# First attention pair: a bias scanned on two partitions and spread by TensorE, loads in three parts, the full scan behind the first logits, ten products before the work

## The reference

```python
# q, k, v: (4, 8, 576, 64); s: (4, 8, 576)
scores = scale * q @ k.T                        # scale = 1/8
s_pos = np.maximum(s, 0.0)
cum = np.cumsum(s_pos, axis=-1)
bias = -(cum[..., :, None] - cum[..., None, :])
scores = np.where(causal, -1e9, scores + np.minimum(bias, 0.0))
attn = softmax(scores);  x = attn @ v           # (2304, 512)
x = ((x @ w_in) * cos(x @ w_in)) @ w_out        # d_ff 2048
out = gated block of rms_norm(x)                # d_ff 1536
```

## Time and profile before

| | us |
|---|---|
| median of 3 runs | 1067.96 (1067.79 to 1068.59) |
| the profiled execution, its own time | 1068.27 |
| its span in the trace | 1066.5 |
| PE busy | 1047.6 (98%) |
| DVE busy | 590.5 (55%) |
| ACT busy | 484.3 (45%) |
| POOL busy | 274.3 (26%) |

### The profile page before, as it was taken

The page is one execution under the profiler, slowest core; times in us unless marked ns, Lnnn a source line. Parts: engine busy times, 40 slices in busy tenths (PEclk is TensorE's granted clock), DMA queues, the critical chain, the costliest instruction groups (busy, mean ns, idle before and its releaser), DMA issues.

```text
span 1066.5 us, 16586 instructions
## 1 busy us (share of the span) xinstructions
PE 1047.6 (98%) x6116; PEld 996.7 (93%) x6116; DVE 590.5 (55%) x1148; ACT 484.3 (45%) x1030; POOL 274.3 (26%) x216
## 2 busy tenths in 40 slices
PE   5999999999999999999999999999999999999998
PEld 4998999899999999999999999999999999999997
DVE  6888888698555655556567644334334334433322
ACT  5888887655554555545546422222222222322211
POOL 5898896575000000000042794000000000000000
PEclk9999999999999999999999999999999999999999
DMA  6654542143000000000011241000000000000000
GB/s 205 200 183 140 170 154 94 54 133 114 2 1 1 1 1 0 0 0 0 0 48 32 89 119 40 30 1 1 30 0 0 30 0 0 30 0 0 30 1 30
DMA packets 23368, 52.35 MB, mean 49 GB/s; under 512 B 3920, under 2 KB 3920, under 8 KB 23312
## 3 DMA queue, kind: packets, MB, share of 16 engines
q1 hardware_dynamic: 23312, 51.62, 15.1%
HBM read 46.74 MB, written 4.87 MB: 48 GB/s over the span
## 4 chain that ended last, share of the span: by engine, by line
PE 93%; DVE 4%; ACT 1%; DMA 1%; issue 1%; POOL 0%; SPq 0%; DVEq 0%; ACTq 0%; POOLq 0%
PE psum L1231 28%; PE psum L1215 17%; PE psum L1155 16%; PE psum L1257 14%; PE psum L1105 7%; PE psum L1136 5%; PE psum L1118 4%; DVE b_r L789 1%; PE psum L1109 1%; DVE b_r L786 1%; DMA raw<-in_qkv 1%; DVE b_lo L827 0%; DVE b_g L822 0%; DVE w L867 0%; DVE first_sq L839 0%
## 5 line engine op out<-in xcount | busy, mean ns | idle before, releaser
L1231 PE MATMUL psum<-c_x,cw 128*128 128x384 f32 x1728 | 313.1, 335 | 0.0
L1231 PEld LDWEIGHTS psum<-c_x,cw 128*128 128x128 f32 x1728 | 303.3, 188 | 6.1
L1215 PE MATMUL psum<-b_hi,w 128*128 128x384 f32 x768 | 211.0, 335 | 4.1 <-DVE b_lo L827 4.1
L1215 PEld LDWEIGHTS psum<-b_hi,w 128*128 128x128 f32 x768 | 140.0, 188 | 5.2 <-DVE b_lo L827 5.0
L929 DVE TENSOR_TENSOR c_t<-psum,c_t 128x384 f32<-128x384 f32 x72 | 40.1, 557 | 186.6 <-ACT c_t L673 186.1
L1257 PE MATMUL psum<-cw,c_hi 128*128 128x512 f32 x432 | 136.2, 396 | 0.1
L673 ACT ACTIVATE c_t<-psum 128x384 f32<-128x384 f32 x72 | 35.4, 492 | 207.4 <-PE psum L1231 206.1
L1215 PE MATMUL psum<-b_lo,w 128*128 128x384 f32 x384 | 128.3, 334 | 0.0
L1105 PE MATMUL psum<-qk 128*128 128x192 f32 (+6 forms) x480 | 99.4, 337 | 11.3 <-DVE qk L716 8.8
L1155 PE MATMUL psum<-bx_even,w 128*128 128x384 f32 x576 | 108.0, 335 | 0.0
L1155 PE MATMUL psum<-bx_odd,w 128*128 128x384 f32 x576 | 107.5, 334 | 0.0
(11 more groups left out here) (92 smaller groups left out, 1473.3 us busy)
## 6 DMA issues: line engine op xcount, KB each, us to landing
raw<-in_qkv SPq DMA_DIRECT2D x15, 864.0 KB, 4.4
stage<-in_w_out SPq DMA_DIRECT2D x28, 256.0 KB, 2.6
raw<-in_qkv SPq DMA_DIRECT2D x16, 320.0 KB, 3.2
inv_row<-inv_rows SPq DMA_DIRECT2D x32, 144.0 KB, 3.4
out<-stage SPq DMA_DIRECT2D x18, 256.0 KB, 2.1
cum<-cum_rows SPq DMA_DIRECT2D x30, 144.0 KB, 3.2
stage<-in_w_in SPq DMA_DIRECT2D x16, 256.0 KB, 2.7
stage<-in_w_gate SPq DMA_DIRECT2D x12, 256.0 KB, 2.6
```

The source lines that it names most:

```text
L1215: last = mm(Y_BANKS[f][:, 0:TB], out1_w(j, a)[:, cols], g[j % 2][:], start=(j == 0 and m == 0), stop=(j == NJ - 1 and m == 2))
L1231: last = mm(to[:, 0:TC], weights(c, a)[:, kc], c_x[:, b, kc], start=(kc == 0 and m == 0), stop=(kc == KC - 1 and m == 2))
```

## The change

The bias of pair 0 is no longer broadcast by DMA. ScalarE's queue loads the two rows of `s` onto two partitions and then all of `s`. VectorE clips and scans the two rows there, into `x_part[0:2]`. GpSimd makes one more constant, `spread` (2 x 128, row 0 is one in columns 0 to 63, row 1 in 64 to 127), in three more instructions. TensorE multiplies `spread` by the scanned rows in two float32 products of 288 columns, so that all 128 partitions have their head's row, and ScalarE copies that from PSUM to `cum8[0]`.

Pair 0 is loaded and split in three parts of 704, 384 and 640 columns, pair 1 in two of 832 and 896. The v of pair 0 is loaded behind pair 1. On VectorE the casts of the constants come before the bias; the full scan and the third low split stand behind the logits of tile 0. TensorE begins with ten 128-column products of ones that nothing reads.

```diff
+FIRST_QK = [0, SEQ + P, SEQ + 4 * P, QK_COLS]
+FIRST_TILES = [0, 1, 4]
+SECOND_QK = SEQ + 2 * P
+WARM_UP = 10
-        CONSTS_POOL = 9
+        CONSTS_POOL = 12
# SP queue
-            for a in range(2):
-                sp.dma_start(cum8[1][HALF_ROWS[a], :], s_h[a:a + 1, :].to_broadcast([64, SEQ])).then_inc(s_first_loaded, 16)
-            for n, (lo, hi) in enumerate(((0, FIRST_QK), (FIRST_QK, QK_COLS), (QK_COLS, PAIR_COLS))):
+            for n in range(3):
+                lo, hi = FIRST_QK[n:n + 2]
                 sp.dma_start(raw[0][:, lo:hi], qkv[0, :, lo:hi]).then_inc(first_loaded[n], 16)
-            sp.dma_start(s_sb[:], s_h).then_inc(s_loaded, 16)
-            load_qk(1)
+            sp.dma_start(raw[1][:, 0:SECOND_QK], qkv[1, :, 0:SECOND_QK]).then_inc(second_loaded, 16)
+            sp.dma_start(raw[1][:, SECOND_QK:QK_COLS], qkv[1, :, SECOND_QK:QK_COLS]).then_inc(qk_loaded[1], 16)
+            sp.dma_start(raw[0][:, QK_COLS:PAIR_COLS], qkv[0, :, QK_COLS:PAIR_COLS]).then_inc(first_v_loaded, 16)
             load_v(1)
# ScalarE
+            act.dma_start(cum8[1][0:2, :], s_h[0:2, :]).then_inc(s_first_loaded, 16)
+            act.dma_start(s_sb[:], s_h).then_inc(s_loaded, 16)
             first_split_hi(0)
             first_split_hi(1)
+            act.wait_ge(first_spread, 1)
+            nc.scalar.copy(cum8[0][:, :].rearrange("p (a n) -> p a n", a=2),
+                           psum[:, 2:4, 0:HALF8]).then_inc(first_cum, 1)
+            first_split_hi(2)
# VectorE: the scan on 128 partitions before the casts goes, and behind the casts stands
+            dve.wait_ge(s_first_loaded, 16)
+            nc.vector.tensor_scalar(cum8[1][0:2, :], cum8[1][0:2, :], 0.0, 1.0 / SCORE_SCALE, ALU.max, ALU.mult).then_inc(first_pos, 1)
+            dve.wait_ge(first_pos, 1)
+            nc.vector.tensor_tensor_scan(x_part[0:2, :], ones_f[0:2, 0:1].to_broadcast([2, SEQ]), cum8[1][0:2, :], 0.0,
+                                         ALU.mult, ALU.add).then_inc(first_scan, 1)
             first_split_lo(0)
             first_split_lo(1)
             dve.wait_ge(s_loaded, 16)
             nc.vector.tensor_scalar(s_sb[:], s_sb[:], 0.0, 1.0 / SCORE_SCALE, ALU.max, ALU.mult).then_inc(spos_ready, 1)
-            dve.wait_ge(spos_ready, 1)
-            nc.vector.tensor_tensor_scan(cum[:], ...).then_inc(cum_ready, 1)
             dve.wait_ge(first_cum, 1)
...
                 do(0, logits, 0)
+                if t == 0:
+                    all_cum()                    # the same scan
+                    first_split_lo(2)
# GpSimd: pair 1 in two parts
+                parts = ((0, SECOND_QK), (SECOND_QK, QK_COLS)) if p == 1 else ((0, QK_COLS),)
# TensorE
+            pe.wait_ge(consts_dve, 1)
+            for _ in range(WARM_UP):
+                mm(bank[7][:, 0:P], ones_f[:], ones_f[:], start=True, stop=True)
             pe.wait_ge(consts_pool, CONSTS_POOL)
             pe.wait_ge(consts_dve, CONSTS_DVE)
+            pe.wait_ge(first_scan, 1)
+            for a in range(2):
+                last = mm(bank[2 + a][:, 0:HALF8], spread[:], x_part[0:2, a * HALF8:(a + 1) * HALF8], start=True, stop=True)
+            last.then_inc(first_spread, 1)
```

More of the change, by code:

```diff
@@ L120, in fused_kernel @@
                 ident = sb("ident", [P, P], F32, sA)
+                spread = sb("spread", [2, P], F32, sA)
                 ident_b = sb("ident_b", [P, P], BF16, sA)
@@ L204, in fused_kernel @@
         first_loaded = [sem(f"first_loaded{i}") for i in range(3)]
+        first_v_loaded = sem("first_v_loaded")
+        second_loaded = sem("second_loaded")
+        first_scan = sem("first_scan")
+        first_spread = sem("first_spread")
         first_hi = sem("first_hi")
@@ L388, in load_qk @@
                 if p == 2:
-                    sp.wait_ge(first_lo, 2)
+                    sp.wait_ge(first_lo, 3)
                 elif p > 2:
-                    at_least(sp, qk_lo, p - 2)
+                    at_least(sp, qk_lo, p - 1)
                 sp.dma_start(raw[p % 2][:, 0:QK_COLS], qkv[p, :, 0:QK_COLS]).then_inc(qk_loaded[p % 2], 16)
@@ L403, in load_cum @@
                 else:
-                    sp.wait_ge(first_cum, 1)
+                    sp.wait_ge(first_scan, 1)
                 for a in range(2):
@@ L712, in first_split_lo @@
             def first_split_lo(n):
-                lo, hi = ((0, FIRST_QK), (FIRST_QK, QK_COLS))[n]
+                lo, hi = FIRST_QK[n:n + 2]
                 at_least(dve, first_hi, n + 1)
@@ L722, in _, with all_cum @@
             nc.vector.tensor_scalar(s_sb[:], s_sb[:], 0.0, 1.0 / SCORE_SCALE, ALU.max, ALU.mult).then_inc(spos_ready, 1)
-            dve.wait_ge(spos_ready, 1)
-            nc.vector.tensor_tensor_scan(cum[:], ones_f[0:NH, 0:1].to_broadcast([NH, SEQ]), s_sb[:], 0.0,
-                                         ALU.mult, ALU.add).then_inc(cum_ready, 1)
             dve.wait_ge(first_cum, 1)
+            def all_cum():
+                dve.wait_ge(spos_ready, 1)
+                nc.vector.tensor_tensor_scan(cum[:], ones_f[0:NH, 0:1].to_broadcast([NH, SEQ]), s_sb[:], 0.0,
+                                             ALU.mult, ALU.add).then_inc(cum_ready, 1)
             def logits(p, n):
@@ L969, in _ @@
                                           pattern=[[-1, P]], channel_multiplier=1))
+            const(nc.gpsimd.memset(spread[:], 1.0))
+            const(nc.gpsimd.affine_select(out=spread[:], in_=spread[:], compare_op=ALU.is_ge, fill=0.0, base=0,
+                                          pattern=[[1, P]], channel_multiplier=-HD))
+            const(nc.gpsimd.affine_select(out=spread[:], in_=spread[:], compare_op=ALU.is_ge, fill=0.0, base=HD - 1,
+                                          pattern=[[-1, P]], channel_multiplier=HD))
             for i in range(0, QT, 2):
@@ L977, in split_qk @@
                 b = p % 2
[L978 to L985, removed]
+                parts = ((0, SECOND_QK), (SECOND_QK, QK_COLS)) if p == 1 else ((0, QK_COLS),)
+                for n, (lo, hi) in enumerate(parts):
+                    if p == 1 and n == 0:
+                        pool.wait_ge(second_loaded, 16)
+                    else:
+                        at_least(pool, qk_loaded[b], 16 * ((p + 1) // 2))
+                    if p >= 2:
+                        at_least(pool, scores_done, QT * (p - 1))
+                    nc.gpsimd.tensor_scalar(qk[b][:, 0, lo:hi], raw[b][:, lo:hi], 1.0, 0.0,
+                                            ALU.mult, ALU.add).then_inc(qk_hi, 1)
+                    at_least(pool, qk_hi, p + 1 if p > 1 else n + 1)
+                    nc.gpsimd.tensor_tensor(qk[b][:, 1, lo:hi], raw[b][:, lo:hi], qk[b][:, 0, lo:hi].bitcast(F32),
+                                            ALU.subtract).then_inc(qk_lo, 1)
             def split_v(p):
@@ L990, in split_v @@
                 if p == 0:
-                    at_least(pool, first_loaded[2], 16)
+                    at_least(pool, first_v_loaded, 16)
                 else:
@@ L1085, in _ @@
             mm = nc.tensor.matmul
+            pe.wait_ge(consts_dve, 1)
+            for _ in range(WARM_UP):
+                mm(bank[7][:, 0:P], ones_f[:], ones_f[:], start=True, stop=True)
             pe.wait_ge(consts_pool, CONSTS_POOL)
             pe.wait_ge(consts_dve, CONSTS_DVE)
+            pe.wait_ge(first_scan, 1)
+            for a in range(2):
+                last = mm(bank[2 + a][:, 0:HALF8], spread[:], x_part[0:2, a * HALF8:(a + 1) * HALF8], start=True, stop=True)
+            last.then_inc(first_spread, 1)
             def scores(p, n):
                 i = TILE[n]
[L1094 to L1097, removed]
+                if p == 0 and n in FIRST_TILES:
+                    pe.wait_ge(first_lo, FIRST_TILES.index(n) + 1)
+                elif p == 1 and n in (0, 2):
+                    pe.wait_ge(qk_lo, 1 if n == 0 else 2)
+                elif p > 1 and n == 0:
+                    pe.wait_ge(qk_lo, p + 1)
                 at_least(pe, logits_ready, QT * p + (n - 1 if n >= 2 else n))
```

8 lines of the change are left out of this document (1 added, 7 removed).

## The result

The changed kernel took 1071.08 us (median of 9 executions, 1070.52 to 1072.66), the kernel before 1068.98 us (9 executions, 1067.79 to 1071.07). The ratio is 1.0021, 95% interval 1.0011 to 1.0031: about 2.1 us slower. The forecast of 1067.1 and its range up to 1069.6 were both missed, on the slow side. The profiled execution took 1070.56 us with a span of 1068.5, against 1068.27 and 1066.5: 2.0 of the 2.3 us lie inside the span. The kernel before had 1067.96 as its median of three when the forecast was made, and 1068.98 here, so 1.0 of the 4.0 us between forecast and result lies in the base.

The account below looks back on a forecast made before the run. VectorE's list, not TensorE's products, was taken to pace the opening. Of 2.2 us gained at tile 1's logits, waits beside GpSimd take back 2.0; with the clock 0.9 us is left, giving 1067.1 us, range 1065.0 to 1069.6.

Parts of the forecast that it names:

- the turns: Opening: VectorE's two-operand SBUF work and GpSimd's instructions exclude each other; waits of 1.1 + 0.9 us take back 2.0 of 2.2.
- two-row scan: Opening, VectorE: the scan of pair 0's two bias rows would be done at 6.65, against 6.77 before.
- the spread: Opening, TensorE: two float32 products of 288 columns would take 1.2 us at 2.4 GHz, 2.2 us at 1.2.
- Tile 0's logits: Opening, pair 0: they would start at 9.0 to 9.3 us, against 11.81 before.
- pair 1 landed late enough: Opening loads: pair 1's first part was taken to land at 7.8 us, between 7.1 at full rate and 8.5.
- I take them to leave it at 2.4 GHz: Opening, TensorE: the ten unread products, about as long as the earlier work before the high clock, would leave it at 2.4 GHz.
- tile 3's logits: Opening, pair 0: with products of tiles 2 and 3 done sooner, they would start at 15.7 to 15.9 against 16.75.
- Rival C: Clock falls to 1.2 GHz in TensorE's stop behind tiles 1 and 2, 11.3 to 14.9; 1068.0 to 1068.9 us, chance 0.10.
- a shift of the logits there is passed on by the waits to the end: After the opening: any shift reaches the end unchanged, since pairs, weights and stores all wait for events of attention.
- the one-input clip of `s`: Opening, VectorE: no row showed GpSimd holding it; if held, the sum stays at -0.9 us, without it -3.2.
- the number of partitions does not show in it: VectorE's scan: 1.36 us on 2 partitions as on 128, an estimate, since only columns count in an instruction's length.

Follow-up runs that it names:

- the repeat: The changed kernel run again with no edit, for a second profile; 1070.87 us, ratio 1.0022 against the kernel before.
- the last one: The changed kernel with 15 unread products at the start, 3 behind tile 0, 12 behind tile 2, GpSimd not held back; 1068.43 us, ratio 0.9996.

## Why the prediction was wrong

**Right: the turns.** The term that the prediction called decisive came as it was worked out. Forecast: scan ready at 10.0 and done at 12.4, GpSimd's high split to 13.3, third split to 14.1, logits of tile 1 at 14.15. Measured: 10.13, 12.48, 13.21, 13.87, 13.81. The two-row scan ended at 6.73 (6.65), the spread took 1.20 (1.2). Tile 0's logits came at 9.44, a little behind the 9.0 to 9.3. Holding GpSimd back brought the lengths to 1.34 and 0.79, as the turns say. It was the right reading of the earlier trace rows. That pair 1 landed late enough for it was partly luck: GpSimd was released at 8.34 in this profile, and between 6.90 and 7.99 in the others without a hold, below 7.3 in two of them.

**Wrong: "I take them to leave it at 2.4 GHz".** This is the step that failed in the opening. Of the forecast gain of 0.9 us some 0.7 came from the clock behind tile 1, and the clock was low from 8.8 to 19.0. The ten products did raise it (the spread took 1.20 us); it did not stay. The forecast for tile 3's logits still came nearly true (15.99 for 15.7 to 15.9), but by luck, as two errors cancel: tile 1's were 0.34 us early, and from there to tile 3's, which waited 0.96 us for TensorE, it took 2.18 us, where the profile with hold and 15 products at full clock has 1.61. The larger price was paid behind it, where tiles run without stops: 5.55 us instead of 4.06 to pair 1's products. The opening ends 0.73 us late instead of 0.9 early, a miss of 1.6. Rival C had the mechanism, and put it behind tiles 1 and 2 only and at 1 in 10. The fall came earlier, behind the ten products and the 1.25 us stop that follows them, and tiles 1 and 3 with their stops of 1.07 and 1.13 us ran at the low clock too. Its forecast of 1068.0 to 1068.9 comes near the opening alone: 1067.96 + 0.73 is 1068.7.

The evidence was in the earlier trace rows: before, TensorE had worked from 12.60 and was at the high clock by 16.51, but with steady work behind it. The prediction carried over the length of that work and not what followed it. Fifteen products move the fall to 14.7, and unread products in the stops do away with it in the profiles of the kernels that have them.

**Missing: the late fall.** No step of the prediction looked past the opening: "a shift of the logits there is passed on by the waits to the end". The stop of 1.9 us at 555 us was in the trace of before, at full clock. Filled, it gave back 1.7 us by the ratios. It is the larger half of the 2.0 us in the profile (1.55 against 0.44) and brings the result outside the range: with the opening's 0.73 us alone it would have been 1068.7 by the base of the forecast, and 1069.7, at its edge, by the base measured beside it.

**How the terms of the change stand.** The scan behind the logits, next to a GpSimd that now starts at 8 us: 2.2 us slower than ahead of them, which includes the late stretch: by the mean clocks all executions with the one have it, and some four of eleven with the other (0.994 or 0.995). The ten products: worth 1.9 us in the changed kernel, nothing measurable in the kernel before. GpSimd's early start: 2.7 us, by the hold. These do not add up, since each moves the others' stops.

**What stays open.** The mean clocks of all 18 executions of the changed kernel agree with a late fall, those of the kernel before in 14 of 88, and other openings lie between: none in the profile with the scan back, one in the profile with hold and 15 products. The stop at 555 us is equally long in both kernels, and the shift does not settle it either: the products behind the stop start at 557.57 in the repeat, with a fall, and at 557.60 in the profile with 15 products, without one. By what way the opening bears on a fall half a millisecond later was not found, and that it does so is seen here as a frequency only. Why ten products raised the clock before the spread in some executions and not in others is open too.

**Two-input work and the clip.** The prediction weighed the Trainium skill, "SBUF — State Buffer", section "SBUF: two separate sides". For instructions with two SBUF inputs this case's traces agree: 2.35 against 1.34 us for the scan, 1.47 against 0.79 for the split. What the prediction had to leave open, the one-input clip of `s`, is shown by two experiments: 2.21 us without unread products and 2.22 in the last one, against 0.44, beside GpSimd's subtraction.

## What to carry to other kernels

Starting one engine's work earlier is no gain if it takes turns with the engine that sets the pace: price each piece of VectorE's critical list with GpSimd's piece ahead of it, and if that is dear, hold GpSimd back by a wait on the last critical piece. After every change of an opening, sum the granted clock over all stretches, far behind the opening too, and look for TensorE's stops. A few unread products in a stop can be worth more than the change, but only as many as end before the next work: six of them delayed tile 3's products by 0.4 us, and 15 at the start ran to 7.34 us in one profile and delayed the spread by as much. An extra product ahead of the work is worth only as much as the stops behind it let it keep.

## What the runs showed of the hardware

- The clock fell while TensorE was busy: from 6.88 to 9.3 us it worked without a stop, and the granted clock went to 0.50 at about 8.8 and stayed there for 10.2 us. What went before was 4.50 us of products and 1.25 us of standing still. It rose at 19.0, when the tiles ran without long stops from about 15. In the other openings with a recorded fall it came at 9.4, 14.7, 8.3 and 8.0 us and lasted 10.2, 3.4, 6.8 and 6.8 us.
- Ten unread products, 4.6 us of work, left TensorE at 2.4 GHz in the repeat (spread 1.20 us) and at 1.2 GHz in the profiles with the hold and with the late stop filled (2.25 us), with the same code ahead of them.
- A fall also followed a stop of 1.9 us in the middle of steady work at full clock (at about 558 us), in some executions and not in others of the same kernel. It lasted 3.4 us and cost 1.55. In the four profiles that have it, it began 0.1 to 1.4 us after TensorE had resumed.
- The column of the granted clock reads 1.00 before its first recorded change, also where TensorE was at 1.2 GHz: in the kernel without unread products it reads 1.00 while the spread takes 2.25 us. Lengths of like products are the better witness. The Trainium skill, "TensorE: Matmul & The Clock Gate", section "Seeing it yourself", warns that the trace's clock events are unreliable; these rows agree.
- The scan of 576 columns takes 1.34 us on 2 partitions, 1.34 on 32 and 1.36 on 128: the number of partitions does not show in it, as the prediction assumed.
- The logits, with one operand from PSUM, ran through GpSimd's subtraction unharmed (0.76 us at 9.44, and 0.76 in the run with the hold, where GpSimd stood still), while the scan and the split beside GpSimd, with both operands in SBUF, waited.
- The first part of pair 1 released GpSimd between 6.90 and 8.34 us in eight profiles with the same loads and no hold, and that moves the order of turns.
